# A Fourier and two-layer kernel: the second sequence's second and third transforms split by even and odd rows

## Time and profile before

| | us |
|---|---|
| median of 3 runs | 948.46 |
| the three runs | 948.46, 934.04, 949.15 |
| the profiled execution's own time | 928.23 |
| its span, first to last instruction | 926.3 |
| TensorE matmul busy (4034 records) | 920.9 |
| VectorE busy | 625.9 |
| GpSimd busy | 573.4 |
| ScalarE busy | 561.3 |

### The profile page before, as it was taken

How to read it: one execution, slowest core, us unless ns; L and a number is a source line. 1 busy time by engine, 2 the same in 40 slices (tenths; PEclk the granted TensorE clock), 3 DMA queues, 4 the chain that set the end, 5 groups by cost and what they waited for, 6 DMA issues and landing times.

```text
span 926.3 us, 11845 instructions
## 1 busy us (share of the span) xinstructions
PE 920.9 (99%) x4034; PEld 757.8 (82%) x4034; DVE 625.9 (68%) x964; ACT 561.3 (61%) x873; POOL 573.4 (62%) x408
## 2 busy tenths in 40 slices
PE   9999999999999999999999999999999999999998
PEld 4688888778888888888888888888888888888886
DVE  5877799464544544544877777787787777777774
ACT  4677666557668666676765555565555555555554
POOL 0477655337877867676697477566647756764443
PEclk9999999999999999999999999999999999999999
DMA  9510200002110220100400200020020002001001
GB/s 354 231 56 24 90 1 1 1 1 90 45 46 23 70 66 1 45 1 1 136 1 1 90 1 1 1 89 1 1 90 1 0 1 90 1 1 44 1 1 45
DMA packets 19825, 40.35 MB, mean 44 GB/s; under 512 B 1802, under 2 KB 15668, under 8 KB 18740
## 3 DMA queue, kind: packets, MB, share of 16 engines
q1 hardware_dynamic: 18980, 39.05, 12.0%
q10 hardware_dynamic: 688, 0.52, 0.2%
q0 software_dynamic: 96, 0.02, 0.0%
HBM read 27.22 MB, written 12.37 MB: 43 GB/s over the span
## 4 chain that ended last, share of the span: by engine, by line
PE 99%; ACT 0%; DVE 0%; issue 0%
PE ps L363 13%; PE ps L365 13%; PE ps L364 13%; PE ps L626 9%; PE ps L630 9%; PE ps L627 9%; PE ps L688 9%; PE ps L684 9%; PE ps L685 9%; PE ps L571 2%; PE ps L527 2%; PE ps L556 1%; PE ps L552 1%; PE ps L694 0%; PE ps L543 0%; ACT out_sb L998 0%
## 5 line engine op out<-in xcount | busy, mean ns | idle before, releaser
L1410 POOL TENSOR_TENSOR gl<-g,gh 128x502 fp32r<-128x502 f32 x192 | 224.8, 1177 | 173.4 <-ACT gh L906 173.3
L1388 POOL TENSOR_TENSOR gl<-g_sb,gh 128x1004 fp32r<-128x1004 f32 x96 | 207.9, 2165 | 134.2 <-ACT g_sb L863 133.8
L900 ACT ACTIVATE g<-ps 128x502 f32<-128x502 f32 x192 | 112.0, 592 | 109.8 <-DVE ps L1267 104.9
L1218 DVE SCALAR_TENSOR_TENSOR h_sb<-n_all,a,ps 128x502 f32<-128x502 f32 x96 | 70.7, 736 | 140.9 <-ACT v_sb L927 140.6
L860 ACT ACTIVATE gh<-h_sb 128x1004 fp32r<-128x1004 f32 x96 | 100.6, 1048 | 90.1 <-DVE h_sb L1223 90.1
L1274 DVE SCALAR_TENSOR_TENSOR g<-g,less_alpha,ps 128x502 f32<-128x502 f32 x192 | 132.7, 732 | 32.7 <-ACT g L900 32.7
L626 PE MATMUL ps<-gh,wo 128*128 128x502 f32 x384 | 148.6, 387 | 0.0
L627 PE MATMUL ps<-gh,wo 128*128 128x502 f32 x384 | 147.4, 384 | 0.0
L685 PE MATMUL ps<-gh,wo 128*128 128x502 f32 x382 | 147.2, 385 | 0.0
L684 PE MATMUL ps<-gh,wo 128*128 128x502 f32 x382 | 147.2, 385 | 0.0
L906 ACT CAST gh<-g 128x502 fp32r<-128x502 f32 x192 | 113.0, 614 | 40.3 <-DVE g L1274 38.6
(11 more groups left out here) (137 smaller groups left out, 1583.0 us busy)
## 6 DMA issues: line engine op xcount, KB each, us to landing
x_tile<-x_tiles SPq DMA_DIRECT2D x6, 1024.0 KB, 13.4
x_rows<-x SPq DMA_DIRECT2D x6, 1004.0 KB, 5.9
out_t<-out_sb SPq DMA_DIRECT2D x11, 502.0 KB, 3.2
x_raw_b<-x_rows SPq DMA_DIRECT2D x18, 251.0 KB, 4.2
stage<-moe_w_out SPq DMA_DIRECT2D x16, 256.0 KB, 4.1
n_parts<-n_rows SPq DMA_DIRECT2D x5, 502.0 KB, 3.5
stage<-moe_w_in SPq DMA_DIRECT2D x8, 256.0 KB, 3.5
w_sb<-moe_w_in SPq DMA_DIRECT2D x3, 512.0 KB, 8.7
```

The lines of the kernel that those rows point to most:

```text
L1388: pool.tensor_tensor(gl[g % 2][:, :, :], g_sb[g % 2][:, :, :], gh[g % 2][:, :, :].bitcast(F32), ALU.subtract).then_inc(gl_done, 1)
L1410: pool.tensor_tensor(gl4[:, k, :], g4[:, k, :], gh4[:, k, :].bitcast(F32), ALU.subtract).then_inc(gl_done, 1)
```

## The change

Blocks 2 and 3 are put in a new order of frequencies: first k up to a quarter of the sequence, then the mirrored k. For a mirrored pair the even rows contribute the same and the odd rows the negative (or the reverse, for one of them). So for sequence 1 TensorE makes only the first half of the columns (188, or 189 with padding), once over the even rows (E) and once over the odd rows (O), and VectorE makes both halves as E + O and E - O. Sequence 0 and the n job use the reordered tables as before.

- Instead of "t2" and "t3" there are four jobs, "t2p", "t2q", "t3p", "t3q"; the jobs stand behind steps 32 to 37 and not 33 to 36. Each has 4 f32 matmuls: E from tile 0 and rows 0 to 63 of tile 1, O from rows 64 to 127 of tile 1 and tile 2.
- ScalarE copies O to `o_sb`, VectorE does 2 or 3 sums into `pq_raw`, ScalarE rounds from there in the next step, and VectorE writes the remainder one step later.
- `n_hold_round` moves from step 37 to 40, and `n_hold_low` from 38 to 41. `W_STEP` moves by 2. `add_n` stays where it is.

```diff
-JOB_AFTER = {1: "n", 33: "t1p", 34: "t1q", 35: "t2", 36: "t3"}
+JOB_AFTER = {1: "n", 32: "t1p", 33: "t1q", 34: "t2p", 35: "t2q", 36: "t3p", 37: "t3q"}
...
-        W_STEP = [41, 57]
+        W_STEP = [43, 59]
...
+            def transform23_parted(blk, s):
+                sb, w = (t2_sb, BLOCK_W[2]) if blk == 2 else (t3_sb, BLOCK_W[3])
+                half, h = w * (s == "q"), w // 2
+                m = {2: (3, 0), 3: (1, 2)}[blk][s == "q"]
+                for o, parts in ((0, ((0, 0, P), (1, 0, P // 2))), (1, ((1, P // 2, P), (2, 0, P)))):
+                    dst = ps[:, e_bank(1, s, blk) + o, 0:h]
+                    for i, (q, r0, r1) in enumerate(parts):
+                        ins = pe.matmul(dst, op_b[QT + q][r0:r1, m, :], sb[r0:r1, q, half:half + h],
+                                        start=i == 0, stop=i == 1)
+                ins.then_inc(t_pe, 1)
...
+            def t23_parted_round(blk, s):
+                act.wait_ge(t1_sum, t1_of(blk, 1, s))
+                for c, o, a, w in cut(BLOCK_AT[blk], BLOCK_W[blk]):
+                    m = 2 * (s == "q")
+                    ins = act.copy(pq[:, 3 + c, m, o:o + w], pq_raw[:, 3 + c, m + 1, o:o + w])
+                ins.then_inc(t23_hi, 1)
...
-                elif former == "t3":
+                elif former != "n":
+                    t23_parted_round(int(former[1]), former[2])
+                if JOB_AFTER.get(g - 3) == "t3q":
                     n_hold_round()
...
+            def t23_sums(blk, s):
+                dve.wait_ge(o_done, t1_of(blk, 1, s))
+                h, m = BLOCK_W[blk] // 2, 2 * (s == "q") + 1
+                for half in range(2):
+                    for c, o, a, w in cut(BLOCK_AT[blk] + half * h, h):
+                        E, O = ps[:, e_bank(1, s, blk), a:a + w], o_sb[:, "pq".index(s), a:a + w]
+                        if half and (blk, s) == (3, "q"):
+                            E, O = O, E
+                        ins = dve.tensor_tensor(pq_raw[:, 3 + c, m, o:o + w], E, O, (ALU.add, ALU.subtract)[half])
+                ins.then_inc(t1_sum, 1)
...
-                elif former == "t3":
+                elif former != "n":
+                    t23_parted_low(int(former[1]), former[2])
+                if JOB_AFTER.get(g - 4) == "t3q":
                     n_hold_low()
```

More of the change, by code:

```diff
@@ L19 @@
 NT = QT * BATCH
-BLOCK_K = [list(range(1, S2, 4)), [S2 - k for k in range(1, S2, 4)], list(range(2, S2, 4)), list(range(0, S2 + 1, 4))]
+BLOCK_K = [list(range(1, S2, 4)), [S2 - k for k in range(1, S2, 4)], [*range(2, S4, 4), *(S2 - k for k in range(2, S4, 4))],
+           [*range(0, S4 + 1, 4), *(S2 - k for k in range(0, S4, 4))]]
 BLOCK_W = [len(k) + len(k) % 2 for k in BLOCK_K]
@@ L267, in build @@
                   (1, 1, "p"), (1, 1, "q"), (2, 1, "p"), (2, 1, "q"), (3, 1, "p"), (3, 1, "q")]
-        T1_JOBS = [j for j in T_JOBS if j[0] == 1]
+        T1_JOBS = [j for j in T_JOBS if j[0] == 1 or j[1] == 1]
         T23_JOBS = [j for j in T_JOBS if j[0] > 1] + ["n_hold"]
@@ L310, in t_bank, with e_bank @@
                 return {1: 1, 2: 4, 3: 6}[blk] + (2 if blk == 1 else 1) * (s == "q")
[L311 to L316, removed]
+            return pair_at(f"t{blk}{s}") + 1
+        def e_bank(b, s, blk=1):
+            return t_bank(blk, b, s) - 1
         A2_BANK, N0_BANK = 7, 2
@@ L329, in turn_free @@
                 pe.wait_ge(t23_lo, t23_of(3, None, "n"))
[L330 to L334, removed]
+            elif isinstance(former, str):
+                pe.wait_ge(t1_sum, t1_of(int(former[1]), 1, former[2]))
+                pe.wait_ge(o_done, t1_of(int(former[1]), 1, former[2]))
             else:
@@ L472, in _ @@
             store_x1(0)
-            sp.wait_ge(t1_lo, len(T1_JOBS))
-            sp.wait_ge(t1_late, len(T1_JOBS))
+            sp.wait_ge(t1_lo, 2 * BATCH)
+            sp.wait_ge(t1_late, 2 * BATCH)
             sp.wait_ge(t23_lo, len(T23_JOBS))
@@ L587, in job @@
                     pe.wait_ge(fold, fold_at(NT - 1) + FOLDS)
-                    for s in "pq":
-                        transform23(int(name[1]), 1, s)
+                    transform23_parted(int(name[1]), name[2])
             def first1(g):
@@ L777, in middle2, with t1_copy @@
                 act.copy(op_b[t][:, 0, 0:1], nfold3[:, 3, NT + t:NT + t + 1]).then_inc(middle_in, 1)
-            def t1_copy(b, s):
-                act.wait_ge(t_pe, t_pe_of(1, b, s))
+            def t1_copy(b, s, blk=1):
+                act.wait_ge(t_pe, t_pe_of(blk, b, s))
                 if b:
-                    act.wait_ge(t1_sum, 2)
-                O = ps[:, t_bank(1, b, s), 0:T1W]
-                if s == "q":
+                    act.wait_ge(t1_sum, t1_of(blk, b, s) - 2)
+                w = BLOCK_W[blk] // (1 if blk == 1 else 2)
+                O = ps[:, t_bank(blk, b, s), 0:w]
+                if s == "q" and blk == 1:
                     act.activation(o_sb[:, 2, :], O, ACT.Identity, scale=n_sign[:, 0:1])
-                act.copy(o_sb[:, "pq".index(s), :], O).then_inc(o_done, 1)
+                act.copy(o_sb[:, "pq".index(s), 0:w], O).then_inc(o_done, 1)
             def t1_round(b, s):
@@ L946, in _ @@
                     t23_round(3, None, "n")
[L947 to L952, removed]
+                elif turn:
+                    t1_copy(1, turn[2], int(turn[1]))
+                former = JOB_AFTER.get(g - 1, "n")
                 if former in ("t1p", "t1q"):
@@ L1140, in t1_sums, with t23_parted_low @@
                 ins.then_inc(t1_sum, 1)
+            def t23_sums(blk, s):
[8 more added lines that the diff above has]
+                ins.then_inc(t1_sum, 1)
+            def t23_parted_low(blk, s):
+                dve.wait_ge(t23_hi, t23_of(blk, 1, s))
+                for c, o, a, w in cut(BLOCK_AT[blk], BLOCK_W[blk]):
+                    m = 2 * (s == "q")
+                    ins = dve.tensor_tensor(pq[:, 3 + c, m + 1, o:o + w], pq_raw[:, 3 + c, m + 1, o:o + w],
+                                            pq[:, 3 + c, m, o:o + w].bitcast(F32), ALU.subtract)
+                ins.then_inc(t23_lo, 1)
             def t1_low(b, s):
@@ L1237, in _ @@
                     t1_sums(1, turn[2])
[L1238 to L1241, removed]
+                elif turn:
+                    t23_sums(int(turn[1]), turn[2])
+                former = JOB_AFTER.get(g - 2, "n")
                 if former in ("t1p", "t1q"):
```

## The result

| | before | changed |
|---|---|---|
| median of 22 runs, us | 931.94 | 934.71 |
| lowest and highest, us | 927.66, 949.78 | 931.56, 963.7 |
| median of the 15 runs of each that the ratio counts, us | 928.14 | 933.79 |
| ratio, 95% interval | | 1.005, 1.003 to 1.007 |

So the change costs 0.5%: some 5 us by the ratio, 5.6 us by the medians of the third row. Some executions of both kernels take 20 us or more longer than the rest, the changed kernel's profiled one among them (span 952.8 us), and ratios leave these out, while some that take about 6 us longer stay in and can put a ratio 0.1 to 0.2% off that of the medians.

A forecast was written before the change was run, and what follows sets the result against it. TensorE was taken to bound the kernel: 928.23 - 0.8 (columns less height changes) + 4.5 (wait for the n row) = 931.9 us profiled, 952 us on the median; range 932 to 957 us.

The forecast's parts named there:

- What bounds the kernel: Whole kernel: TensorE, busy 920.9 of 926.3 us, so only its own work and its waits change the time.
- The n row: Step 43: n row three steps later, so add_n(3) delays gl(41) and TensorE waits 4.2 to 5.0 us, 4.5 taken.
- the 4.7 and the 1.6 us: Slack before: 4.7 us in SyncE's chain for the load, 1.6 us between the end of gl(41) and its reader.
- The short records: The four jobs: 32 records of 188 or 189 columns at 0.160 us replace 24 at 0.317, saving 2.5 us.
- The half-height matmuls: The four jobs: two height changes each at 0.21 us, 1.7 us lost, leaving 0.8 us saved.
- lower and upper 64 rows at the same time: The four jobs: both halves of the array might overlap, at most 1.3 us more saved, counted only in the range.
- both rules: The four jobs: changing tiling mode drains TensorE, tiles work independently; first alone 0.8 us saved, with the second some 2.
- VectorE and ScalarE: Steps 32 to 39: extra sums and copies fit; tightest place, h behind "t1q", passes with 0.3 us; no cost taken.
- The clock: Behind TensorE's pause: a rival said the clock falls, 3 us more, 935 us, on the median 955; chance 0.18.
- likeliest case: Step 43: TensorE waits 4 to 5 us, less 0.8 to 2.5 us of saved columns; chance 0.6.
- The rival's 3 us: Behind the pause: cost of a fall to 1.2 GHz, from some 6 us of slow weight loads at the start; chance 0.18.
- The number: Whole kernel: 931.9 us for the profiled execution, 0.4% more; factor 1.004 on the median 948.46 gives 952 us.

The follow-up runs named there:

- full-height run: Changed kernel with add_n(3) behind gl(42) and the half-height matmuls reading all 128 rows: 924.9 us in one run, 927.25 for before.
- three and four steps late: Kernel before with only the n row's rounding and remainder three or four steps later (W_STEP 2 or 3): 935.04 us, ratio 1.006; 938.32 us, one run.
- filling the pause: Changed kernel plus 18 matmuls that nothing reads, ahead of the wait for gl(41): 931.01 us, ratio 1.0024; without them 933.75 us, 1.0053.

## Why the prediction was right or wrong

*What bounds the kernel.* Right: each microsecond that TensorE won or waited appears in the time.

*The n row.* Right in place, cause and size. Forecast: `add_n(3)` waits 6.5 to 7.3 us, measured 7.3; the load is issued 2.7 us after the remainder, measured 2.69; TensorE waits 4.2 to 5.0 us with 4.5 taken, measured 4.6. The landing sat at the far end, 4.2 us, as said for a load with the transfers of an x chunk behind it. One sentence of it is short: beside the 4.7 and the 1.6 us there were 0.8 us ahead of `gl(41)`, so the slack was 7.1 us and not 6.3; the sum by points of time had them.

*The short records.* Right: 0.160 us each, not bounded by their weight load. The full-height run gives 1.28 us for eight.

*The half-height matmuls.* The price of a change was right, but a term was left out of the sum. A change costs 0.20 us where the rows of line 543 said 0.21. But the prediction took "lower and upper 64 rows at the same time" into the range only, on the ground that no row showed it. It is real, 0.32 us a job, 1.3 us over the four. So the jobs saved 2.0 us and not 0.8. By both rules of the page "TensorEngine Tiling (Array Packing)" of the Trainium skill, section "Key Properties", the prediction had named some 2 us, and that is what the traces show.

*VectorE and ScalarE.* Right: the sums and copies are hidden. The tightest place was the one named, and with a job of 1.36 us it waits 0.2 us, where 0.1 had been given for a job of 1.3.

*The clock.* This is the step that failed. The forecast's likeliest case left the clock at 2.4 GHz through a pause of 4.5 us and gave the fall 0.18. It fell in every profile with such a pause (the changed kernel twice, three and four steps late). By the traces it cost 1.6 to 2.6 us, and filling the pause gave 2.4 us back. The rival's 3 us came from the start of the kernel, where weight loads take 0.34 us though the table of windows has the granted clock at 1.00 there; behind the pause, with the column at 0.50, loads take 0.33 us, which bears that reading out. With the clock the sum for the profiled execution is 928.23 - 2.0 + 4.6 + 2.6 = 933.4 us, the rival's 935 with the columns as measured; the median of the runs that the ratio counts is 933.8.

*The number.* 952 us was the factor 1.004 times a median of three, and here a second step failed, the base. The median of 22 runs of before is 931.94 and not 948.46, so the forecast time was 17 us too high. The profiled execution at 928.23 was the better base; the prediction saw that it lay 2% under its median and didn't weigh it. The sign and the late n row held. That the factor 1.004 came so near the measured 1.005 is in part luck: 1.2 us too little saved on the columns stood against 2.6 us left out for the clock.

## What to carry to other kernels

When a step is moved, write down everything that hangs on its last semaphore, through the DMA queue and the other engines, and count each consumer's slack in steps: here 12 us of delay met 7 us of slack, and the consumer stood in order ahead of work that TensorE wanted. Price a pause of TensorE with what comes behind it, not with its length alone: 4.6 us of waiting cost up to 7.2 here. Put matmuls of half height next to each other on opposite halves of the array, so that the change into half height and the change out of it are paid once and the halves overlap (1.36 us a job against 2.06).

## What the runs showed of the hardware

- A pause of TensorE of 0.7 us left the granted clock at 1.00; pauses of 4.4 to 7.6 us brought it to 0.50. It stayed there for 3.1 to 5.3 us after work went on, which cost 1.6 to 2.6 us; with a pause of 7.6 us it was 3.7 us, so the loss did not grow with the pause in the one run that had it. With the pause filled to 0.5 us the clock stayed at 1.00.
- Two f32 matmuls of 64 rows on opposite halves of the array took the time of one (0.52 us against 0.51, the change included). A change between 128 and 64 rows cost 0.20 us each way.
- A one-row VectorE operation between buffers outside PSUM took 1.79 us beside a running GpSimd operation and ended 0.4 us after it, and took 0.53 us with GpSimd idle. The changed kernel shows the slow form with 128 rows too, in the remainder at 202.95: 1.80 us for 378 columns.
